# Softmax sums and their inverses in a PSUM bank instead of SBUF

## The reference

```
q, k, v: [8 batches, 8 heads, 576, 64]
k_p, v_p = mean of k, v over groups of 8 rows            # 72 keys per head
scores = q @ k_p.T / sqrt(64);  scores -= max over keys
attn = exp(scores);  attn = attn / (sum over keys + 1e-9)
x = attn @ v_p                                           # as [4608 tokens, 512]
h = x @ w_in;   g = h if h >= 1, 0 if h <= -1, else (h + 1)**2 / 4;   x = g @ w_out
h = x @ w_in2;  out = relu(h)**2 @ w_out2
```

## Time and profile before

| | |
|---|---|
| median of 3 runs | 1597.81 us (1596.72 to 1598.21) |
| the profiled execution | 1594.51 us |
| its span, first to last instruction | 1592.7 us |
| PE busy | 1569.9 us (99%) |
| DVE busy | 1140.2 us (72%) |
| ACT busy | 833.5 us (52%) |
| POOL busy | 249.8 us (16%) |
| DMA engines busy, 7 to 28.5 us | 101% of their share, 319 GB/s |

### The profile page before, as it was taken

How to read it: one execution, slowest core, us unless ns; L and a number is a source line. 1 busy time by engine, 2 the same in 40 slices (tenths; PEclk the granted TensorE clock), 3 DMA queues, 4 the chain that set the end, 5 groups by cost and what they waited for, 6 DMA issues and landing times.

```text
span 1592.7 us, 25304 instructions
## 1 busy us (share of the span) xinstructions
PE 1569.9 (99%) x9216; PEld 1553.6 (98%) x9216; DVE 1140.2 (72%) x1763; ACT 833.5 (52%) x1444; POOL 249.8 (16%) x353
## 2 busy tenths in 40 slices
PE   6999999999999999999999999999999999999999
PEld 5899999999999999999999999999999999999999
DVE  8766667666655768768778877666667987876874
ACT  4766567766666734444435654434455643443442
POOL 6636437916510000000000000000000000000000
PEclk9999999999999999999999999999999999999999
DMA  8366559657635652453452733443447645246241
GB/s 279 98 208 233 186 189 310 224 181 235 222 137 174 211 185 79 144 185 96 129 177 81 268 139 134 140 139 120 157 151 257 217 159 170 81 146 193 73 132 40
DMA packets 174460, 265.92 MB, mean 167 GB/s; under 512 B 15616, under 2 KB 152832, under 8 KB 174336
## 3 DMA queue, kind: packets, MB, share of 16 engines
q1 hardware_dynamic: 174336, 264.30, 49.9%
HBM read 157.29 MB, written 106.95 MB: 166 GB/s over the span
## 4 chain that ended last, share of the span: by engine, by line
PE 93%; DVE 4%; issue 1%; ACT 1%; POOL 1%; DMA 0%; DVEq 0%; ACTq 0%; POOLq 0%
PE bank L772 42%; PE bank L662 24%; PE bank L795 22%; PE bank L629 2%; PE bank L639 1%; PE bank L640 1%; DVE gf L1175 1%; DVE b L1168 1%; PE bank L654 1%; PE bank L651 1%; PE bank L652 1%; PE bank L653 1%; DVE total L1113 0%; DVE f_lo L1143 0%; DVE total L1111 0%
## 5 line engine op out<-in xcount | busy, mean ns | idle before, releaser
L772 PE MATMUL bank<-gf,f_hi 128*128 128x384 f32 x2688 | 682.6, 334 | 0.4 <-DVE u_b L1185 0.3
L772 PEld LDWEIGHTS bank<-gf,f_hi 128*128 128x128 f32 x2688 | 485.2, 188 | 1.2 <-DVE u_b L1185 0.7
L772 PE MATMUL bank<-gf,f_lo 128*128 128x384 f32 x1344 | 448.9, 334 | 0.0
L895 ACT ACTIVATE gf<-b 128x768 fp32r<-128x768 f32 x336 | 278.5, 845 | 264.3 <-PE bank L772 177.0
L1175 DVE TENSOR_TENSOR gf<-b,gf 128x768 fp32r<-128x768 f32 x336 | 314.5, 952 | 43.3 <-ACT gf L895 43.3
L795 PE MATMUL bank<-xf,w_hi 128*128 128x384 f32 x1344 | 340.9, 334 | 0.0
L662 PE MATMUL bank<-x_hi,wi_hi 128*128 128x384 f32 x768 | 265.8, 346 | 2.8 <-DVE g_st L1256 2.8
L662 PE MATMUL bank<-x_hi,wi_lo 128*128 128x384 f32 x768 | 257.3, 335 | 0.0
L662 PE MATMUL bank<-x_lo,wi_hi 128*128 128x384 f32 x768 | 257.3, 335 | 0.0
L772 PEld LDWEIGHTS bank<-gf,f_lo 128*128 128x128 f32 x1344 | 252.3, 188 | 0.0
L795 PEld LDWEIGHTS bank<-xf,w_hi 128*128 128x128 f32 x1344 | 242.4, 188 | 0.0
(11 more groups left out here) (92 smaller groups left out, 1497.2 us busy)
## 6 DMA issues: line engine op xcount, KB each, us to landing
b<-g_dram SPq DMA_DIRECT2D x192, 384.0 KB, 4.2
g_dram<-g_st SPq DMA_DIRECT2D x192, 192.0 KB, 2.0
g_dram<-c_st SPq DMA_DIRECT2D x192, 192.0 KB, 1.9
s_dram<-su_s SPq DMA_DIRECT2D x24, 512.0 KB, 2.8
k_raw<-k SPq DMA_DIRECT2D x32, 288.0 KB, 3.5
q_sb<-q SPq DMA_DIRECT2D x48, 192.0 KB, 2.9
y_dram<-o_st SPq DMA_DIRECT2D x48, 192.0 KB, 1.9
x_raw<-y_dram SPq DMA_DIRECT2D x24, 384.0 KB, 5.1
```

Of the source, the lines that this page charges most:

```text
L772: last = mm(dst[:, 0:H], w[:, 2 * i + kt, cols], x[:, half, kt, :], start=q_ < 3 and i == 0 and kt == 0 and h == 0, stop=q_ >= 4 and i == ...
L895: copy(gf[layer][r % GRING][:, 0], unit_source(n)[:, 2 * i:2 * i + 2, :], ACT.Copy).then_inc(gf_hi, 1)
```

## The change

`total` and `share` are no longer SBUF tiles. There are now two of each, one in each scores bank, in columns that the scores leave free: columns 432 to 437 for `total`, 440 to 445 for `share`. Unit a uses those of bank `a % 2`. The instructions, their order, their sizes and their waits are as before; three of the four in `normal` now read or write PSUM with one of their operands or both, and L1119 reads `prob` from SBUF and `share` from PSUM.

```diff
-        total = at("total", 216.125, [P, 2 * NT])
-        share = at("share", 216.1875, [P, 2 * NT])
...
+        total, share = ([s[:, NT * KEYS + n:NT * KEYS + n + 2 * NT] for s in s_ps] for n in (0, 8))
...
-                vec.tensor_reduce(total[:, :], probs, AX_X, ALU.add).then_inc(s_total, 1)
+                vec.tensor_reduce(total[a % 2], probs, AX_X, ALU.add).then_inc(s_total, 1)
                 dve.wait_ge(s_total, a + 1)
-                vec.tensor_scalar(total[:, :], total[:, :], 1e-9, None, ALU.add).then_inc(s_eps, 1)
+                vec.tensor_scalar(total[a % 2], total[a % 2], 1e-9, None, ALU.add).then_inc(s_eps, 1)
                 dve.wait_ge(s_eps, a + 1)
...
-                vec.reciprocal(share[:, :], total[:, :]).then_inc(s_share, 1)
+                vec.reciprocal(share[a % 2], total[a % 2]).then_inc(s_share, 1)
                 dve.wait_ge(s_share, a + 1)
-                vec.tensor_tensor(probs, probs, share[:, :].unsqueeze(2).broadcast_to([P, 2 * NT, G]), ALU.mult)\
+                vec.tensor_tensor(probs, probs, share[a % 2].unsqueeze(2).broadcast_to([P, 2 * NT, G]), ALU.mult)\
                     .then_inc(s_prob, 1)
```

## The result

| | before | after |
|---|---|---|
| median | 1597.26 us (1596.26 to 1598.29, 6 runs) | 1588.8 us (1588.36 to 1589.07, 6 runs) |
| profiled execution, its span | 1594.51, 1592.7 us | 1589.07, 1587.3 us |

The ratio is 0.9948 (95% interval 0.9938 to 0.9958), a gain of 8.5 us between the medians. The spans are worth a look of their own: 1587.9 was forecast and 1587.3 measured. The medians differ by more than the two profiled executions do, by 8.5 against 5.4 us, and the runs of the kernel after lie closer together (0.7 against 2.0 us). Both turn out to be the point of this case.

A forecast was written before the change was run, and what follows sets the result against it. PE was taken as the bound, busy 1569.9 of 1592.7 us. The terms 1.25 + 0.48 + 1.3 + 1.8 - 0.04 gave 4.8 us, taken off the median 1597.81 for 1593.0 us, range 1591.8 to 1594.3.

The forecast's parts named there:

- The exclusion: L1113 and L1119 on DVE and POOL's instructions exclude each other; with PSUM operands both always take their medians, 172 and 609 ns.
- Rival B: The change frees only L1113, while L1119 still excludes POOL; gain 2.5 us, 1595.3 us, chance 0.10.
- rival E: Nothing moves, because some unseen wait sets PE's start; 1597.8 us, chance 0.05.
- The price of PSUM: Reading or writing six numbers in PSUM adds 0.01 us per instruction of `normal`, 0.04 per unit, bounded -0.01 to +0.06 each.
- Rival D: Slower because PSUM writes are dear; at 0.2 us more per instruction of `normal`, 1608.4 us; chance 0.05.
- Step (1): `normal(4)`, on DVE straight before L1256: stalls of L1113 and L1119 go, L1256 moves up by 1.25 us.
- Step (4): Start-up chain up to `normal(4)`: DVE and POOL lose stalls and waits, so `normal(4)` comes 1.8 us earlier.
- fixed point: Start-up: batch 2's values land at 19.49 us behind a full DMA queue, so POOL still starts them at 19.57.
- rival C: The batch-2 landing isn't fixed: 1.3 us sooner, POOL follows DVE; gain 5.8 us, 1592.0 us, chance 0.08.
- rival A: The start-up gain gets lost because something taken as covered becomes last; gain 3.0 us, 1594.8 us, chance 0.12.
- Step (2): `normal(5)`, before the transposes at 55.34 us: the wait on L1119 goes, PE gains 0.48 us.
- Step (3): After 57 us: five weight-load waits of 2.1 us go, less 0.16 us each, a gain of 1.3 us.

The follow-up runs named there:

- share_only: The changed kernel's move for the inverses alone: `share` in PSUM, `total` in one SBUF tile; 1592.01 us, ratio 0.9972 to the kernel before.
- total_only: The changed kernel's move for the sums alone: `total` in PSUM, `share` in one SBUF tile; 1591.25 us, ratio 0.9962 to the kernel before.
- changed: The changed kernel run and profiled again with no edit; 1589.12 us, ratio 0.9949 to the kernel before.
- same: The kernel before, run and profiled again with no edit; 1597.19 us, ratio 1.0, span 1593.2 us.
- same_c: The kernel before, profiled once more with no edit; 1596.28 us, span 1594.5 us.
- same_b: The kernel before, profiled once more with no edit; 1598.23 us, span 1596.4 us.
- v_sooner: The changed kernel with the batch-2 loads issued ahead of two weight loads; 1588.76 us, ratio 0.9953 to the kernel before.

## Why the forecast was right in its mechanism and wrong in its size

**The exclusion: right, shown.** Both instructions are free in `after`; one tile at a time frees one each. Why the small add in SBUF is held and the reciprocal isn't stays open. Rival B (only L1113 is freed) falls by `share_only`, rival E by the result.

**The price of PSUM: right.** 16 ns per unit, where I took 40 and bounded -40 to 240. Writing a result there cost 8 ns (the sum; the reciprocal in `share_only`), reading an operand there 6 (the reciprocal in `total_only`), both together 13 at most, and L1119 is 5 ns quicker. Rival D needed 125 ns per instruction. The figures of the Trainium skill ("VectorE: DVE Perf Modes", the TRN2 errata), 65 ns more per instruction that reads PSUM, are not borne out by the durations here: where the source alone moved they changed by +6 and -5 ns, and all four instructions together show 16.

**Steps (1) and (4), up to the fourth hidden step: right.** I had 1.25 + 1.8 = 3.05 us. The mean start over four profiles of the kernel before is 43.25, over the two of the one after 40.30: 2.95. Step (1) can be read alone, from the start of `normal(4)` to the fourth hidden step: 4.10 us in `before` (39.64 to 43.74), 2.86 in `after` (37.19 to 40.05), so 1.24 against my 1.25. DVE's rows of `before`, then `after`:

```profile
39.64 0.59 DVE L1111 TENSOR_REDUCE total<-prob 128x6 f32<-128x432 f32 x1
```
```profile
37.19 0.60 DVE L1111 TENSOR_REDUCE bank<-prob 128x6 f32<-128x432 f32 x1
```

Step (4), the start of `normal(4)`, has 1.71 us in the means against my 1.8. On the very pair of profiles that I forecast it has 2.45, because the landing was no fixed point there: POOL started batch 2 at 18.72 instead of 19.57, and `v_bd` came 2.45 us sooner than 34.95, in `changed` with its landing at 19.46 1.95 sooner (`after`, then `changed`):

```profile
32.50 0.94 POOL L535 TENSOR_TENSOR v_bd<-v_pool,mask 128x256 f32<-128x256 f32 x1
```
```profile
33.00 0.94 POOL L535 TENSOR_TENSOR v_bd<-v_pool,mask 128x256 f32<-128x256 f32 x1
```

In `same` and `same_c` POOL even started batch 2 at 18.95 and 18.86 without a wait. So rival C holds in part: the landing moves, and where it came sooner, or was made to, POOL met L1136 next. That the sum met the means to 0.1 us is in part luck, as one landing stood for all. No sign of rival A.

**Step (2): right.** From the fourth hidden step to the transposes of unit 5 it took 11.60 us (43.74 to 55.34) and takes 11.15 (40.05 to 51.20), 0.45 against my 0.48.

**Missing: a term between the fourth hidden step and S6.** S6 came at 56.37 us in the mean of the four profiles before and at 52.10 in the two after (51.85, 52.34), 4.3 us sooner; (1), (2) and (4) give 3.5. The lower clock in two of the four accounts for the 0.8 between them: from the fourth hidden step to S6 `same_b` and `same_c` took 1.1 and 2.4 us more than the 12.25 of the other two, 0.9 in the mean of four. In the profile that I read it was not there at all.

**Step (3) failed as a size.** "After 57 us the five weight-load waits of 2.1 us go", 1.3 us. On that execution it is right: span minus S6 was 1536.65 us and is 1535.45, 1.2 less. Over the executions it isn't. The other three of before have 1538.13, 1539.35 and 1537.20, a mean of 1537.8 with the first, and `after` and `changed` 1535.2: 2.6 us, twice my term. The rule behind the term was right: the weight-load waits less 0.16 us for each give 1.3, 2.7, 4.0 and 1.5 us in the four profiles, 2.4 in the mean. What failed is that one execution's waits stood for all.

**The step from a span to a median failed, and this cost the most.** I wrote "The median of runs lies 3.3 us above that execution; I take the difference off the median". That holds only if the 3.3 us have nothing to do with what the change removes. They consisted in good part of it: more of DVE's stalls behind POOL reached PE in the slots, 1.3 us in the mean, and the lower clock behind the fourth hidden step cost 0.9. The kernel after shows neither in its two profiles, and its median lies on its profiled execution (1588.8 and 1589.07 us). The forecast of that execution, 1589.7, was 0.6 us off; adding the 3.3 us back made it 1593.0. The four profiles before have a mean span of 1594.2, 6.9 above that of after (2.95 + 0.45 + 0.9 + 2.6), so they account for 6.9 of the 8.5 us. The last 1.6 us lie in executions that were timed and not profiled, and stay open. A part may be chance: four profiles are few, and over all runs the medians are 1596.86 (67 runs) and 1588.86 (11), 8.0 apart.

The spread was the sign that I passed by. The runs before spanned 1.5 us with only three of them, and all lay over 2 us above the profiled one.

## What to carry to other kernels

Look at the maximum of a line beside its median before looking at the mean: an instruction on six numbers with 172 ns at the median and 1214 at most is not slow, it is locked out, and moving its small operands to PSUM can cost 16 ns per unit and win 8 us in all. Where timed runs lie above the profiled one, profile the kernel again before pricing a change: if what makes them longer is what the change removes, the gain is larger than in that profile, and the new median can land on its own profiled time, as it did here. A race that two engines decide anew each time costs a different amount in each execution; and a transfer that holds a chain can have a second such race right behind it.

## What of the hardware was not expected

- Reading one small operand from PSUM made the 128x432 multiplication 4 to 5 ns quicker (604 against 608 and 609 ns); the reciprocal of six numbers took 197 ns reading PSUM, 199 writing it and 204 doing both, against 191 in SBUF.
- POOL loses as DVE does: L525 took 1.71 instead of 1.26 us in `v_sooner` beside a DVE instruction with two SBUF inputs. Its busy time fell by 5.2 us though nothing of it was touched.
- In three of nine profiles with a PE wait of 2.8 to 3.0 us before the fourth hidden step the granted clock fell to half, at the end of the wait or within 1 us behind it, and stayed there for some 3 to 7 us; the same wait, made on purpose in the changed kernel, did not do it in three profiles. Earlier in the start-up the clock fell in 11 of 17 profiles, in `after` where PE had waited 2.2 us.
- The reciprocal with its input and output in SBUF ran wholly inside POOL instructions in 10 of 48 units and took 193 ns at most, while the small add with the same places was held for up to 1.0 us.
